# Linear attention, SoLU layer and top-2 experts on one core: expert slots split into 25 whole and six half ones

## The chip, the core and the metric

The kernel runs on one core of a Trainium2 chip. Its engines work side by side and wait for each other by semaphores: TensorE (PE, matrix products into the eight PSUM banks), VectorE (DVE), ScalarE (ACT), GpSimd (POOL, here mostly the issuer of indirect DMAs) and SyncE (SP, here the issuer of plain DMAs). The metric is the device time of one execution in microseconds (us), as the median of several runs.

## What is computed

Three stages, one after another, on 3072 tokens (4 batches of 768) with 384 features. This change touches the third only.

```python
attn_out = _attn_ref(q, k, v, a_re, a_im)          # decaying linear attention, 8 heads of 48
x = attn_out.transpose(0, 2, 1, 3).reshape(B * S, H * D)
x = _moe_ref(x, w_in, w_out, g_ln)                 # dense: 384 -> 1024, softmax gating, norm, -> 384
# _moe2_ref: E = 8 experts, each token goes to its two best
noisy_logits = x @ w_gate + np.log1p(np.exp(x @ w_noise)) * noise
top2, top2_w = two_largest(noisy_logits), softmax_of_the_two
for e in range(E):
    for k in range(2):
        mask = top2[:, k] == e
        h = np.maximum(x[mask] @ w1[e], 0.0)       # 384 -> 1024
        out[mask] += top2_w[mask, k, None] * (h @ w2[e])   # 1024 -> 384
```

## The kernel before

Up to about 600 us the first two stages run, tile by tile of 128 tokens, with the routing at their end. It writes the rows of x to `xs` in DRAM, and for each of the 6144 pairs (token, expert) a tag (row number, weight) to `tags`, sorted by expert: expert e has a region of its own.

The third stage works in **slots**. A slot is 256 rows of one expert (`CAP = 256`, two units of 128, `SUB = 2`). The number of slots is fixed when the program is built, `SLOTS = 31`, the most that eight experts can need. A small table, made on DVE in 14 chained steps while the last tags are written, says for each slot its expert and its first tag row (`slot_expert`, `slot_row`). A slot that gets no rows still does all its work on the engines, and its gathers and scatters move nothing.

Every product is made of three, from a high and a low part of both factors (`split_product`). So weights and tokens are first split: ACT casts the high part (`w1h`, `w2h`, `sxh`, `hh`), DVE subtracts it from the value for the low part (`w1l`, `w2l`, `sxl`, `hl`).

What a slot does, in the order that is written out for each engine, `s` being the slot:

- SP: `load_mine` (the tags of slot s + 3), then `load_w1` and `load_w2` (1.5 MB each, for slot s + 1) into the single buffers `raw1` and `raw2`. A load waits until DVE has made the low parts of the weights before it.
- POOL: `gather` (two indirect DMAs, the tokens of slot s + 2 into `xg`), `partial` (two more, the rows of `out` so far into `prev`), `give` (two more, the new rows into `out`). `partial` of a slot waits until the scatter of the slot before has landed.
- PE: eight blocks f. Each has `expert_hidden` of the next block (nine matmuls, w1 stationary, 256 tokens moving) and `expert_result` of this one (six matmuls, hidden rows stationary, 384 columns of w2 moving, accumulated over the eight blocks in the banks `Y_BANK`). In block 2 stand the six transposes of the next slot's tokens (`tokens`).
- ACT: the relu into `hh` of each block; in blocks 1 to 3 the casts of the next slot's w1 (`w1_piece`, three), in blocks 4 to 7 those of w2 (`w2_piece`, four), in block 4 the tokens.
- DVE: `hl` of each block and the low parts of the same pieces; in block 1 (`GIVE = 1`) the `give` of the slot before, `yo = bank * weight + prev`.

The order within an engine is the order of the program text; nothing reorders it. `apart` and `wait` are waits for semaphores.

Of the kernel before, what the change touches and what calls it, by code (L numbers as in the profile page):

```python
# [32 lines left out]
SLOTS = (2 * NTOK - (E - 1)) // CAP + E  # L33
# [11 lines left out]
LIVE = T - B  # L45
CHAIN = 3 * (LINE - 1)
# [4 lines left out]
LN_LIMIT = math.log(0.999)  # L51

# [35 lines left out]
def solu_moe_program(nc, q, k, v, a_re, a_im, w_in, w_out, g_ln, w_gate, w_noise, noise, w1, w2, out):  # L88
# [3 lines left out]
    with ExitStack() as ctx:  # L92
# [17 lines left out]
        tail_row = keep("tail_row", [1, E], I32)  # L110
        cnt = keep("cnt", [P, 4, E])
# [78 lines left out]
        thresh = m2("thresh", [P, E, MAXS])  # L190
        slot_no = m2("slot_no", [1, SLOTS, E])
        slot_cmp = m2("slot_cmp", [P, SLOTS, E])
        fills = m2("fills", [P, E, MAXS])
        assert m2.at <= early_end
        raw1 = m2("raw1", [P, KC, F])
        raw2 = m2("raw2", [P, FC, DM])
# [14 lines left out]
        prev = [m2(f"prev{i}", [P, SUB, DM]) for i in range(2)]  # L211
        bank = psum("bank", [P, 8, 512])
# [82 lines left out]
        raw1_loaded = sem("raw1_loaded")  # L295
        raw2_loaded = sem("raw2_loaded")
# [8 lines left out]
        h2_mm = sem("h2_mm")  # L305
        hh_done = sem("hh_done")
# [13 lines left out]
        turned = bank[:, 4:6, :].rearrange("p b x -> p (b x)")[:, 0:KC * CAP]  # L320

# [59 lines left out]

        def over_slots(eng, body):

            body(0, 0, True)
            body(1, 1, True)
            with eng.Fori(1, SLOTS // 2) as i:
                body(2 * i, 0, True)
                body(2 * i + 1, 1, True)
            for s in range(SLOTS // 2 * 2, SLOTS):
                body(s, s % 2, s < SLOTS - 1)  # L390
# [24 lines left out]
        def _(sp):  # L415
# [78 lines left out]
            def body(c, b, n):  # L494
# [6 lines left out]
                if n == T:  # L501
                    prepared(sp)
                    sp.dma_start(raw1[:], w1[0:1].rearrange("e (c p) f -> p (e c) f", p=P)).then_inc(raw1_loaded, 16)
                    sp.dma_start(raw2[:], w2[0:1].rearrange("e (c p) d -> p (e c) d", p=P)).then_inc(raw2_loaded, 16)
# [10 lines left out]
            def load_w1(s):  # L515
                e = sp.value_load(slot_expert[0:1, bass.ds(s, 1)], min_val=0, max_val=E - 1)
                apart(sp, (w1_lo, KC * s))
                sp.dma_start(raw1[:], w1[bass.ds(e, 1)].rearrange("e (c p) f -> p (e c) f", p=P)).then_inc(raw1_loaded, 16)

            def load_w2(s):  # L520
                e = sp.value_load(slot_expert[0:1, bass.ds(s, 1)], min_val=0, max_val=E - 1)
                apart(sp, (w2_lo, W2P * s))
                sp.dma_start(raw2[:], w2[bass.ds(e, 1)].rearrange("e (c p) d -> p (e c) d", p=P)).then_inc(raw2_loaded, 16)

            def load_mine(s, k):
                row = sp.value_load(slot_row[0:1, bass.ds(s, 1)], min_val=0, max_val=ROWS - CAP)
                apart(sp, (y_sent, 32 * (s - NM + 1)))
                sp.dma_start(mine[k][:].rearrange("p s i -> p (s i)"),
                             tags[bass.ds(row, CAP)].rearrange("(p s) i -> p (s i)", s=SUB)).then_inc(mine_loaded[k], 16)
# [5 lines left out]
            sp.wait_ge(slot_step, 14)  # L535
# [10 lines left out]
            sp.wait_ge(y_sent, 32 * SLOTS)  # L546
# [3 lines left out]
        def _(pool):  # L550
# [72 lines left out]
            def body(c, b, n):  # L623
# [16 lines left out]
                if n == T:  # L640
# [4 lines left out]
                    nc.gpsimd.iota(slot_no[:], [[1, SLOTS], [0, E]], base=0, channel_multiplier=0,  # L645
                                   allow_small_or_imprecise_dtypes=True).then_inc(tables_ready, 1)
                    nc.gpsimd.iota(thresh[:], [[0, E], [CAP, MAXS]], base=0, channel_multiplier=0,
# [67 lines left out]
        def _(act):  # L715
# [267 lines left out]
            for s_ in range(SLOTS):  # L983
                slot(s_, s_ % 2, s_ < SLOTS - 1)
# [692 lines left out]
```

## Time and profile before

| | us |
|---|---|
| median of 3 runs | 1179.63 (1179.08 to 1182.27) |
| the profiled execution | 1182.65, with a span of 1180.9 |
| mean granted TensorE clock over the span | 0.944 of full speed |

The profile comes from one execution. Its times are counted from the start of its span; the difference between the execution's time and its span lies outside of all engines' work. Start times and durations of single instructions overlap a little where an engine is pipelined: a matmul's duration is about 0.17 us longer than its distance to the next.

### The profile page before, as it was taken

What the parts mean: (1) busy time and instruction counts of PE and PEld (TensorE: products, weight loads), DVE (VectorE), ACT (ScalarE), POOL (GpSimd) and SP (SyncE); (2) the same over time, 40 slices, a digit from 0 to 9 for tenths busy, and PEclk for the clock granted to TensorE, in tenths of its full rate; (3) what the DMA queues carried; (4) which work ended last, traced back from release to release, by engine and by line L of the source; (5) the groups of instructions that cost most, each with busy time, mean ns of one, the idle gap of its engine ahead of it and who ended that gap; (6) DMA issues with size and microseconds to landing.
All of it is one profiled execution on the core that took longest, in us unless ns stands there. A gap on an engine that the chain in (4) does not pass through costs nothing.

```text
span 1180.9 us, 21982 instructions
## 1 busy us (share of the span) xinstructions
PE 1046.8 (89%) x7898; PEld 983.2 (83%) x7898; DVE 857.6 (73%) x1592; ACT 647.9 (55%) x1105; POOL 459.4 (39%) x413
## 2 busy tenths in 40 slices
PE   0467789989999999999939999999999999999996
PEld 0256678877887888888739999999999999999995
DVE  5799788988888899646445777676676676676672
ACT  6733856756756745645524555555555555555551
POOL 4011233344444443434531443453453453454342
PEclk9868888989999999999968999999999999999998
DMA  9430121231221211222216667676676676776740
GB/s 260 152 101 21 41 88 31 65 88 28 68 89 28 68 36 54 49 55 64 98 28 246 230 210 266 237 234 237 229 254 247 238 246 214 237 256 206 231 142 1
DMA packets 85980, 167.51 MB, mean 142 GB/s; under 512 B 18566, under 2 KB 57696, under 8 KB 85872
## 3 DMA queue, kind: packets, MB, share of 16 engines
q1 hardware_dynamic: 72336, 137.61, 36.3%
q0 software_dynamic: 13440, 28.40, 6.5%
q8 instruction: 63, 1.03, 0.4%
q14 instruction: 45, 0.37, 0.1%
q10 hardware_dynamic: 96, 0.10, 0.0%
HBM read 148.83 MB, written 21.92 MB: 145 GB/s over the span
## 4 chain that ended last, share of the span: by engine, by line
PE 59%; DVE 2%; ACT 1%; issue 1%; DMA 1%; POOL 0%; POOLq 0%; DVEq 0%; ACTq 0%; SPq 0%
PE bank L1412 23%; PE bank L1609 22%; PE bank L1473 4%; PE bank L1521 4%; PE bank L1403 3%; PE bank L1495 1%; PE bank L1533 1%; ACT z L943 1%; ACT x2t L938 0%; PE bank L1510 0%; DVE w1l L1145 0%; DMA xg<-xs,mine 0%; DMA tags<-tag,idx 0%; DVE zl L1247 0%; PE bank L1553 0%
## 5 line engine op out<-in xcount | busy, mean ns | idle before, releaser
L975 ACT ACTIVATE hh<-bank 128x256 fp32r<-128x256 f32 x248 | 95.4, 385 | 256.3 <-PE bank L1412 256.3
L1412 PE MATMUL bank<-sxh,w1h 128*128 128x256 f32 x744 | 212.0, 285 | 2.1 <-DVE sxl L1362 2.1
L1412 PE MATMUL bank<-sxh,w1l 128*128 128x256 f32 x744 | 210.3, 283 | 0.0
L1412 PE MATMUL bank<-sxl,w1h 128*128 128x256 f32 x744 | 210.0, 282 | 0.0
L1381 DVE SCALAR_TENSOR_TENSOR hl<-bank,hh 128x256 fp32r<-128x256 f32 x248 | 105.0, 423 | 120.5 <-ACT hh L975 120.5
L697 POOL DMA_INDIRECT out<-yo,mine x62 | 77.5, 1250 | 279.0 <-DVE yo L1374 261.1
L1609 PE MATMUL bank<-w2h,hh 128*128 128x384 f32 x496 | 167.4, 337 | 0.0
L1609 PE MATMUL bank<-w2l,hh 128*128 128x384 f32 x496 | 166.8, 336 | 0.0
L1609 PE MATMUL bank<-w2h,hl 128*128 128x384 f32 x496 | 166.6, 336 | 0.0
L1412 PEld LDWEIGHTS bank<-sxh,w1h 128*128 128x128 f32 x744 | 140.8, 189 | 2.5 <-DVE sxl L1362 2.5
L1412 PEld LDWEIGHTS bank<-sxh,w1l 128*128 128x128 f32 x744 | 141.5, 190 | 0.0
L1412 PEld LDWEIGHTS bank<-sxl,w1h 128*128 128x128 f32 x744 | 141.0, 190 | 0.0
L1151 DVE TENSOR_TENSOR w2l<-raw,w2h 128x768 fp32r<-128x768 f32 x124 | 118.6, 958 | 27.8 <-ACT w2h L785 27.8
L1145 DVE TENSOR_TENSOR w1l<-raw,w1h 128x1024 fp32r<-128x1024 f32 x93 | 113.5, 1222 | 20.0 <-ACT w1h L780 16.7
L785 ACT ACTIVATE w2h<-raw 128x768 fp32r<-128x768 f32 x124 | 103.5, 837 | 0.0
L780 ACT ACTIVATE w1h<-raw 128x1024 fp32r<-128x1024 f32 x93 | 97.6, 1051 | 0.0
L676 POOL DMA_INDIRECT xg<-xs,mine x62 | 86.2, 1391 | 24.5 <-issue 17.4
L1609 PEld LDWEIGHTS bank<-w2h,hh 128*128 128x128 f32 x496 | 94.4, 190 | 0.2 <-DVE hl L1381 0.2
L1609 PEld LDWEIGHTS bank<-w2l,hh 128*128 128x128 f32 x496 | 94.4, 190 | 0.0
L1609 PEld LDWEIGHTS bank<-w2h,hl 128*128 128x128 f32 x496 | 93.4, 188 | 0.0
L1473 PE MATMUL bank<-wi_hi,xh 112*128 112x512 f32 x192 | 83.8, 436 | 5.7 <-issue 5.7
L688 POOL DMA_INDIRECT prev<-out,mine x62 | 74.1, 1195 | 22.1 <-issue 18.3
(202 smaller groups left out, 2328.4 us busy)
## 6 DMA issues: line engine op xcount, KB each, us to landing
raw<-in_w SPq DMA_DIRECT2D x62, 1536.0 KB, 7.6
ar<-in_a_re SPq DMA_DIRECT2D x6, 768.0 KB, 4.7
turn<-in_a_im SPq DMA_DIRECT2D x6, 768.0 KB, 5.9
qk<-in_q SPq DMA_DIRECT2D x48, 96.0 KB, 2.4
qk<-in_k SPq DMA_DIRECT2D x48, 96.0 KB, 2.5
out<-wide SPq DMA_DIRECT2D x9, 512.0 KB, 11.5
vt<-in_v SPq DMA_DIRECT2D x24, 192.0 KB, 2.7
xs<-x SPq DMA_DIRECT2D x24, 192.0 KB, 2.8
```

Of the source, the lines that this page charges most:

```text
L676: nc.gpsimd.indirect_dma_start(xg[par][:, u, :], None, xs, bass.IndirectOffsetOnAxis(ap=mine[k][:, u, 0:1], axis=0), bounds_check=NTOK - 1 ...
L688: nc.gpsimd.indirect_dma_start(prev[par][:, u, :], None, out, bass.IndirectOffsetOnAxis(ap=mine[k][:, u, 0:1], axis=0), bounds_check=NTOK ...
L697: nc.gpsimd.indirect_dma_start(out, bass.IndirectOffsetOnAxis(ap=mine[k][:, u, 0:1], axis=0), yo[par][:, u, :], None, bounds_check=NTOK - ...
L780: nc.scalar.activation(w1h[par][:, cc, :], raw1[:, cc, :], ACT.Copy).then_inc(w1_hi, 1)
L785: nc.scalar.activation(w2h[par][:, W2C * j:W2C * (j + 1), :], raw2[:, W2C * j:W2C * (j + 1), :], ACT.Copy).then_inc(w2_hi, 1)
L975: nc.scalar.activation(hh[:, f % NH, :], bank[:, f % 2, 0:CAP], ACT.Relu).then_inc(hh_done, 1)
L1145: V.tensor_tensor(w1l[par][:, cc, :], raw1[:, cc, :], w1h[par][:, cc, :].bitcast(F32), ALU.subtract).then_inc(w1_lo, 1)
L1151: V.tensor_tensor(w2l[par][:, cut, :], raw2[:, cut, :], w2h[par][:, cut, :].bitcast(F32), ALU.subtract).then_inc(w2_lo, 1)
L1381: V.scalar_tensor_tensor(out=hl[:, f % NH, :], in0=bank[:, f % 2, 0:CAP], scalar=0.0, in1=hh[:, f % NH, :].bitcast(F32), op0=ALU.max, op1= ...
L1412: ins = MM(dst, stationary[a_](cc), moving[b_](cc), start=(n_ == 0), stop=(n_ == len(terms) - 1))
L1473: ins = MM(bank[:, 4 + half, :], (xh, xl)[a_][0:PR, cc, :], (wi_hi, wi_lo)[b_][0:PR, cc, 512 * half:512 * half + 512], start=(k_ % (3 * NP ...
L1609: ins = MM(bank[:, Y_BANK[par] + u, 0:DM], a_[:, f % NH, rows], b_[par][:, f, :], start=(f == 0 and k_ == 0), stop=(f == FC - 1 and k_ == 2))
```

## The change

The slots become 31 again, but of two sizes: 25 whole ones of 256 rows and six half ones of 128 rows, at places 3, 8, 13, 18, 23 and 28 of the list, so that two whole ones end it. An expert takes a whole slot for each 256 rows, another whole one for a rest over 128, and a half one for a rest of up to 128 rows; rests that find no half slot take whole ones from the end. The table gets longer for that, 24 chained steps on DVE and six more small tables (iota) on POOL.

A half slot has another form. Its tokens (128) are the stationary operand and w1 moves in two parts of 512 columns, so that the hidden rows come out one token to a partition; ACT's relu puts them into `row_h`, PE turns them in eight transposes into free banks, ACT and DVE make the high and low parts, and then the results follow, one unit instead of two.

The orders around it change: `raw1` and `raw2` get two buffers each and a load waits for the weights of two slots back; POOL reads `prev` first and then gathers for slot s + 3 instead of s + 2; the w1 pieces for the slot behind a half slot are made at the end of the slot before it; and the give stands in block 4 behind a half slot, then in blocks 3, 2 and 1.

```diff
-SLOTS = (2 * NTOK - (E - 1)) // CAP + E
+WHOLE, HALVES = 25, 6
+SLOTS = WHOLE + HALVES
+HALF_SLOTS = (3, 8, 13, 18, 23, 28)
...
+def give_block(s):
+
+    return max([GIVE] + [4 - (s - t) for t in HALF_SLOTS if t <= s])
...
 SP
             def load_w1(s):
-                apart(sp, (w1_lo, KC * s))
-                sp.dma_start(raw1[:], ...
+                apart(sp, (w1_lo, KC * (s - 1)))
+                sp.dma_start(raw1[s % 2][:], ...
...
 POOL
             for s in range(SLOTS):
-                if s + 2 < SLOTS:
-                    gather(s + 2, s % 2, (s + 2) % NM)
                 partial(s, s % 2, s % NM)
+                if s == 0:
+                    gather(2, 0, 2)
+                if s + 3 < SLOTS:
+                    gather(s + 3, (s + 3) % 2, (s + 3) % NM)
                 give(s, s % 2, s % NM)
...
 ACT, at the end of slot(s)
+                if is_half(s + 1) and s + 2 < SLOTS:
+                    for cc in range(KC):
+                        w1_piece(s + 2, par, cc)
...
+            def half_slot(s, par, more):
+                def row(part):
+                    act.wait_ge(h2_mm, s0 + part + 1)
+                    wait(act, row_turned, k - 1 + part)
+                    nc.scalar.activation(row_h[:, 512 * part:512 * (part + 1)], bank[:, part, :], ACT.Relu).then_inc(row_done, 1)
+                def high(part):
+                    act.wait_ge(row_turned, k + part + 1)
+                    act.wait_ge(y2_mm, s0 - 2 + 2 * part)
+                    nc.scalar.activation(hh_half[:, 4 * part:4 * (part + 1), :] ..., bank[:, turn_bank(par, part), :], ACT.Copy).then_inc(hh_done, 1)
+                row(0)
+                if more:
+                    tokens(s + 1, 1 - par)
+                row(1)
+                high(0)
+                high(1)
+                if more:
+                    for j_ in range(W2P):
+                        w2_piece(s + 1, 1 - par, j_)
...
 DVE
-                    if f == GIVE and s > 0:
+                    if s > 0 and f == give_block(s - 1):
                         give(s - 1, 1 - par, (s - 1) % NM)
...
 PE
+            def half_hidden(s, par, part):
+                if part == 0:
+                    pe.wait_ge(sx_lo, s + 1)
+                    pe.wait_ge(w1_lo, KC * (s + 1))
+                pe.wait_ge(hl_done, steps(s) - 1 + part)
+                cols = slice(512 * part, 512 * (part + 1))
+                split_product(bank[:, part, :],
+                              (lambda cc: sxh[par][:, cc, 0:P], lambda cc: sxl[par][:, cc, 0:P]),
+                              (lambda cc: w1h[par][:, cc, cols], lambda cc: w1l[par][:, cc, cols]), KC, h2_mm)
+            def half_turn(s, par, part):
+                pe.wait_ge(row_done, 2 * HALF_SLOTS.index(s) + part + 1)
+                for k_ in range(4):
+                    turn(bank[:, turn_bank(par, part), k_ * P:(k_ + 1) * P], row_h[:, ...], row_turned if k_ == 3 else None)
...
+            def half_slot(s, par, more):
+                if more:
+                    tokens(s + 1, 1 - par)
+                half_hidden(s, par, 1)
+                half_turn(s, par, 0)
+                half_turn(s, par, 1)
+                if more:
+                    first_hidden(s + 1, 1 - par)
+                half_result(s, par, 0)
+                half_result(s, par, 1)
```

How the instructions stand on DVE at the first half slot (slot 3), between the last block of slot 2 and the second block of slot 4; a name's last number tells buffers apart. Before, from the last two blocks of a slot on:

```order
L1151 TENSOR_TENSOR w2l_147<-raw_143,w2h_146 128x768
L1381 SCALAR_TENSOR_TENSOR hl<-bank,hh 128x256 x2
L1374 SCALAR_TENSOR_TENSOR yo_159<-bank,mine_65,prev_161 128x384 x2
L1145 TENSOR_TENSOR w1l_149<-raw_142,w1h_148 128x1024
L1381 SCALAR_TENSOR_TENSOR hl<-bank,hh 128x256
```

Of the change:

```order
L1236 TENSOR_TENSOR w2l_152<-raw_1_164,w2h_151 128x768
L1230 TENSOR_TENSOR w1l_146<-raw_0_143,w1h_145 128x1024 x3
L1471 TENSOR_TENSOR sxl_155<-bank,sxh_153 128x768
L1483 SCALAR_TENSOR_TENSOR yo_159<-bank,mine_61,prev_161 128x384 x2
L1509 TENSOR_TENSOR hl<-bank,hh 128x512 x2
L1236 TENSOR_TENSOR w2l_148<-raw_0_144,w2h_147 128x768 x4
L1490 SCALAR_TENSOR_TENSOR hl<-bank,hh 128x256 x2
```

Where one piece stood between two blocks, three w1 pieces, the tokens and the give of the slot before now stand in a row ahead of the half slot's two `hl`, and four w2 pieces behind them.

On ACT the same place reads, of the change:

```order
L832 ACTIVATE w2h_151<-raw_1_164 128x768
L827 ACTIVATE w1h_145<-raw_0_143 128x1024 x3
L1047 ACTIVATE row_h<-bank 128x512
L1016 ACTIVATE sxh_153<-bank 128x768
L1047 ACTIVATE row_h<-bank 128x512
L1052 ACTIVATE hh<-bank 128x512 x2
L832 ACTIVATE w2h_147<-raw_0_144 128x768 x4
L1029 ACTIVATE hh<-bank 128x256 x2
```

The three w1 casts stand ahead of the first relu of the half slot, where before one relu and one cast took turns.

On POOL, the last slots. Before:

```order
L676 DMA xg_66<-xs,mine_60 128x384 x2
L688 DMA prev_160<-out,mine_64 128x384 x2
L697 DMA out<-yo_158,mine_64 3072x384 x2
L688 DMA prev_161<-out,mine_65 128x384 x2
L697 DMA out<-yo_159,mine_65 3072x384 x2
L688 DMA prev_160<-out,mine_60 128x384 x2
L697 DMA out<-yo_158,mine_60 3072x384 x2
```

Of the change:

```order
L721 DMA xg_65<-xs,mine_59 128x384 x2
L742 DMA out<-yo_160,mine_62 3072x384 x2
L733 DMA prev_161<-out,mine_63 128x384
L742 DMA out<-yo_159,mine_63 3072x384
L733 DMA prev_162<-out,mine_64 128x384 x2
L742 DMA out<-yo_160,mine_64 3072x384 x2
L733 DMA prev_161<-out,mine_59 128x384 x2
L742 DMA out<-yo_159,mine_59 3072x384 x2
```

The last gather stands one slot earlier, and the third slot from the end moves one unit instead of two.

## Rows read from the trace of the kernel before

**Rows 1.** Busy time by stretches: start:end, length, then busy us (count) of each engine.

```profile
core 0: us, PE busy (x) PEld busy (x) DVE busy (x) ACT busy (x) POOL busy (x), PEclk, DMA share, GB/s
900.00:1000.00 100.00, 100.00 (x718) 99.83 (x718) 70.86 (x104) 54.19 (x92) 42.58 (x34) 1.00 0.71 246
```

**Rows 2.** Chain of waits, expert slots: start us, us, what.

```profile
739.12 1.07 PE bank L1412 x9
...
756.68 1.06 PE bank L1412 x9
...
1151.45 1.07 PE bank L1412 x9
1152.52 1.04 PE bank L1609 x6
1153.57 1.07 PE bank L1412 x9
```

**Rows 3.** Instructions in time, first phase: start, us, engine, line, [idle before, releaser].

```profile
521.75 0.40 PE L1473 MATMUL bank<-wi_lo,xh 112*128 112x512 f32 x1
...
526.74 0.39 PE L1473 MATMUL bank<-wi_hi,xl 112*128 112x512 f32 x1
...
527.17 1.23 DVE L1275 TENSOR_REDUCE nmax<-bank 128x1 f32<-128x1024 f32 x1 [3.26 <-PE bank L1473]
```

**Rows 4.** Groups by shape, 840 to 1120 and (last two) 300 to 560 us.

```profile
L1151 DVE TENSOR_TENSOR w2l<-raw,w2h 128x768 fp32r<-128x768 f32 x64 | 61.3, 958 | 14.8 <-ACT w2h L785 14.8
L1145 DVE TENSOR_TENSOR w1l<-raw,w1h 128x1024 fp32r<-128x1024 f32 x48 | 58.7, 1222 | 10.3 <-ACT w1h L780 8.3
L785 ACT ACTIVATE w2h<-raw 128x768 fp32r<-128x768 f32 x64 | 53.6, 837 | 0.0
L780 ACT ACTIVATE w1h<-raw 128x1024 fp32r<-128x1024 f32 x48 | 50.5, 1052 | 0.0
L1362 DVE TENSOR_TENSOR sxl<-bank,sxh 128x768 fp32r<-128x768 f32 x16 | 15.2, 951 | 0.0
...
L1312 DVE TENSOR_TENSOR xl<-bank,xh 112x512 fp32r<-112x512 f32 x13 | 8.9, 687 | 8.1 <-ACT xh L949 8.1
L949 ACT ACTIVATE xh<-bank 112x512 fp32r<-112x512 f32 x13 | 7.5, 577 | 0.0
```

**Rows 5.** A load of w1, its first cast, and the landing of all w1 loads.

```profile
898.32 0.38 SPq L518 DMA_DIRECT2D raw<-in_w  x1
...
909.11 1.05 ACT L780 ACTIVATE w1h<-raw 128x1024 fp32r<-128x1024 f32 x1
...
DMA to landing us min/median/max: 6.3/7.6/8.5
```

**Rows 6.** From give to give: DVE, POOL, and the landing of the reads of prev.

```profile
892.03 1.13 DVE L1374 SCALAR_TENSOR_TENSOR yo<-bank,mine,prev 128x384 f32<-128x384 f32 x2
...
895.50 1.35 POOL L697 DMA_INDIRECT out<-yo,mine  x1 [0.30 <-issue]
...
1144.61 1.05 POOL L688 DMA_INDIRECT prev<-out,mine  x1 [1.91 <-DMA out<-yo,mine]
...
DMA to landing us min/median/max: 3.9/5.0/5.7
```

**Rows 7.** The last two gives on DVE, of slots 29 and 30.

```profile
1155.43 1.13 DVE L1374 SCALAR_TENSOR_TENSOR yo<-bank,mine,prev 128x384 f32<-128x384 f32 x2
...
1169.60 1.14 DVE L1374 SCALAR_TENSOR_TENSOR yo<-bank,mine,prev 128x384 f32<-128x384 f32 x2 [1.41 <-PE bank L1609]
```

**Rows 8.** Between the phases: the first row lists loaded by table, DVE's first token part.

```profile
613.56 2.92 SPq L528 DMA_DIRECT2D mine<-tags  x3
...
621.77 0.96 DVE L1362 TENSOR_TENSOR sxl<-bank,sxh 128x768 fp32r<-128x768 f32 x1 [10.53 <-ACT sxh L966]
```

**Rows 9.** A pause of PE in the first phase, and the stretch behind it.

```profile
502.56 0.77 PE L1473 MATMUL bank<-wi_hi,xh 112*128 112x512 f32 x1 [1.35 <-issue]
...
502.00:505.70 3.70, 3.13 (x8) 2.52 (x9) 2.80 (x4) 1.51 (x3) 2.21 (x3) 0.55 0.39 24
```

More of the change, by code:

```diff
@@ L45 @@
 LIVE = T - B
+SLOT_STEPS = 24
 CHAIN = 3 * (LINE - 1)
@@ L51, with is_half, table_row, units @@
 LN_LIMIT = math.log(0.999)
+def is_half(s):
+    return s in HALF_SLOTS
+def table_row(s):
+    return WHOLE + HALF_SLOTS.index(s) if is_half(s) else s - sum(t < s for t in HALF_SLOTS)
+def units(s):
+    return 1 if is_half(s) else SUB
+def units_upto(s, step=1):
+    return sum(units(t) for t in range(s, -1, -step))
+def give_block(s):
+    return max([GIVE] + [4 - (s - t) for t in HALF_SLOTS if t <= s])
+def steps(s):
+    return sum(2 if is_half(t) else FC for t in range(s))
 def wait(eng, sem, value):
@@ L211, in solu_moe_program @@
         prev = [m2(f"prev{i}", [P, SUB, DM]) for i in range(2)]
+        raw1.append(m2("raw1_1", [P, KC, F]))
+        raw2.append(m2("raw2_1", [P, FC, DM]))
+        row_h = m2("row_h", [P, F])
         bank = psum("bank", [P, 8, 512])
@@ L674, in gather @@
                 wait(pool, sxt_mm, s - 1)
-                for u in range(SUB):
+                for u in range(units(s)):
                     nc.gpsimd.indirect_dma_start(xg[par][:, u, :], None, xs,
@@ L1337, in _, with over @@
             one = slice(0, 1)
-            count, slots, upto = cnt[:, 0, :], cnt[:, 1, :], cnt[:, 2, :]
+            count, whole, any_, odd, pairs_upto, odd_upto, odd_ahead = (cnt[:, i_, :] for i_ in range(7))
             by_slot = [1, SLOTS, E]
+            def over(x):
+                return x[one].unsqueeze(1).to_broadcast(by_slot)
             then(V.scalar_tensor_tensor(out=count, in0=expert_no[:], scalar=-float(REGION), in1=rank_base[:],
                                         op0=ALU.mult, op1=ALU.add))
-            then(V.tensor_tensor(fills[:], count.unsqueeze(2).to_broadcast([P, E, MAXS]), thresh[:], ALU.is_gt))
@@ L1357, in _ @@
-            then(V.tensor_copy(tail_row[:], rank_base[one]))
+            for i_ in range(2):
+                then(V.tensor_tensor(fills[:, i_], count.unsqueeze(2).to_broadcast([P, E, MAXS]), thresh[:, i_], ALU.is_gt))
+            then(V.tensor_reduce(cnt[:, 1:3, :], fills[:], AX.X, ALU.add))
+            then(V.tensor_tensor(odd, any_, whole, ALU.subtract))
+            then(V.tensor_tensor_scan(pairs_upto, ones[:, 0:E], whole, 0.0, ALU.mult, ALU.add))
+            then(V.tensor_tensor_scan(odd_upto, ones[:, 0:E], odd, 0.0, ALU.mult, ALU.add))
@@ new lines, in _ @@
+            then(V.tensor_tensor(odd_ahead, odd_upto, odd, ALU.subtract))
+            in_pairs, in_odd = (slot_cmp[:, i_] for i_ in range(2))
+            own = in_pairs
+            at_pair, at_odd = (x[:].unsqueeze(2).to_broadcast(by_slot) for x in (pair_no, odd_no))
+            then(V.tensor_tensor(in_pairs, over(pairs_upto), at_pair, ALU.is_le))
+            then(V.tensor_reduce(slot_f[:, 0, :], in_pairs, AX.X, ALU.add))
+            then(V.tensor_tensor(in_pairs, in_pairs, over(whole), ALU.mult))
```

250 lines of the change are left out of this document (163 added, 87 removed).

## The prediction, made before the changed kernel was timed

> **What bounds the kernel now.** I read in this order. First, the busy time by stretches: in 900 to 1000 us TensorE (PE) is busy for all 100 us at the full granted clock, while VectorE (DVE) has 71 us of work, ScalarE (ACT) 54 us and the DMA engines a share of 0.71 [rows 1]. So in the expert phase, about 622 to 1170 us, PE alone sets the pace and a matmul less is time less. Second, the chain of waits. The same block of nine matmuls stands at 739.12 and at 756.68, one slot later: a slot of 256 rows costs **17.56 us**. A hidden block starts at 1151.45 and its result block at 1152.52, the next hidden block at 1153.57: nine matmuls of 256 columns are 1.07 us (0.118 each), six of 384 columns 1.05 us (0.175 each) [rows 2]. Eight such pairs are 16.9 us; the remaining 0.66 us are the six transposes of the next slot's tokens, 0.11 us each. There are 31 such slots, 544 us.
>
> **What a half slot costs PE.** 31 slots stay 31, but six of them hold 128 rows. In a half slot the tokens are the stationary operand and w1 moves 512 columns at a time: 2 parts of 9 matmuls. The only rows of that width are those of the first phase, 22 steps from 521.75 to 526.74, 0.227 us each, with 112 partitions instead of 128 [rows 3]; I take that value, since the columns, not the partitions, should count. 18 x 0.227 = 4.09. The hidden rows must then be turned: 8 transposes x 0.11 = 0.88. The result is 8 blocks of 3 matmuls of 384 columns: 24 x 0.175 = 4.20. Its own tokens: 3 x 0.11 = 0.33. Sum **9.50 us** of PE work, 8.06 less than a whole slot.
>
> **What PE waits for in a half slot.** Take 0 at the start of the first hidden part; this walk uses PE's order of the change. Part 0 ends at 2.04, the last result block of the slot before at 3.09, the next slot's six transposes at 3.75, part 1 at 5.79. Turn 0 needs row_h part 0. ACT does three w1 casts before it (3 x 1.05, and rows overlap by about 0.1) and the copy of 512 columns (0.58) [rows 4]: done near 3.6, 2.2 us before it is wanted. Turn 0 runs 5.79 to 6.23. Turn 1 needs row_h part 1: a reader of a bank starts 0.2 us after PE's last matmul has made way (DVE at 527.17, against 526.74 + 0.23) [rows 3], so ACT runs 5.99 to 6.57, and PE starts at about 6.60: **0.37 us idle**. Turn 1 ends at 7.04, and PE covers with the next slot's first hidden block until 8.10. Meanwhile ACT copies turned part 0 (behind the row, to 7.1) and DVE subtracts it, 0.69 [rows 4], to 7.8; the result needs it at 8.10. Part 1 follows at 7.8 on ACT and 8.5 on DVE; wanted at 10.2. DVE ahead of that has three w1 pieces (1.22 each), the tokens (0.95) and two gives (1.13 together) [rows 4, 6], from about 1.2: free at about 6.9, 0.3 before it is needed. So in total 9.50 + 0.37 = 9.87, and six half slots save 6 x (17.56 - 9.87) = **46.1 us**. The wait is bounded by 0 and by the chain with nothing beside it (0.2 + 0.58 + 0.44 + 0.2 + 0.58 + 0.69 = 2.7, and 0.44 for the other turn: 3.1 us). I take 0.37, the walk, because ACT and DVE are free in it; the bounds are +2.2 and -17 us on the saving.
>
> One rule prices the matmuls otherwise. The Trainium skill ("TensorE: Matmul & The Clock Gate", section Back-to-back issue gap) gives columns divided by 2.4 GHz plus 2.5 ns. By that 512 columns would take 0.216 us, 384 0.163, 256 0.109 and 128 0.056, and the same sum would save about 43 us instead of 46; the rows disagree with it by 5 to 8% (0.227, 0.175, 0.118), and I use the rows.
>
> **The whole slots around.** In the slot before a half one ACT and DVE get three w1 pieces more, at its end, and in the half slot four w2 pieces. Their sum over five slots is unchanged except for turns, and both have slack in a stretch (29 and 46 us in 100) [rows 1]. After the half slot ACT has the four w2 casts (4 x 0.84) behind it before the next relu, and DVE 4 x 0.96 [rows 4]: DVE is through at 12.4, then the first hl block until 12.7; PE wants it at 13.4 (end of the results 12.3, then a hidden block). No price; without this 0.7 us, PE waits for the difference.
>
> **Weights and tokens.** raw1 and raw2 are doubled, so a load waits for the weights two slots back instead of one. Before, w1 is issued at 898.32 and its first cast starts at 909.11, 10.8 us later, and landing takes 6.3 to 8.5 us [rows 5]. Now a pair is asked for a slot earlier, so a half slot's short time is covered. The bytes of weights stay as they are, 31 pairs, in 46 us less: DMA share from 0.71 to about 0.77. Cost nothing; if it did, a cast would be late. Gathers go a slot earlier too and stand behind the read of prev on POOL: no path.
>
> **The chain from one give to the next.** give on DVE, scatter, its landing, read of prev, landing, next give. From the give at 892.03 to the end of the second scatter issue, 895.50 + 1.35, are 4.8 us; the read of prev can start 1.9 us after that (at 1144.61 it waited 1.91 for the scatter), its second issue 1.3 later, and that lands after 5.0 (3.9 to 5.7) [rows 6]: 13.0 us. In the middle gives are 15.4 us apart (17.56 less a block of 2.11): nothing. At the **end** it shows. Two whole slots end the list, and the give of slot 29 moves from block 1 of slot 30 to block 3: 4.2 us later. Today it starts at 1155.43 and the last give at 1169.60, when PE is done [rows 7], 14.2 us later. Now that gap is 14.2 - 4.2 = 10.0 us, and the chain asks for 13.0 (11.9 with the shortest landing): PE is done and the last give waits **2 to 3 us**. I take 2.8.
>
> **Between the phases.** DVE's table is 24 chained steps instead of 14. Before, they end at 611.24, since DVE idles 10.53 us before 621.77 [rows 8]; even with 0.5 us for each of the ten more they end by 616.3: covered. I reckon with 4 us, 615.2. SP waits for the table with the load of the row lists: first such load at 613.56 [rows 8], now about 615.4, and everything behind it on SP (the weights of slot 1) 1.8 us later; slot 1's weights are wanted only behind the first hidden blocks of slot 0. POOL builds six small tables more. All told 0 to 1 us, taken as 0.5.
>
> **Sum.** The profiled execution took 1182.65 us (span 1180.9), the median of the runs is 1179.63, 3.0 lower. 1182.65 - 46.1 + 2.8 + 0.5 = 1139.9; on the scale of the median **1136.8, rounded 1137**, 3.6% faster.
>
> **Rivals.**
> A. The narrow chain stands open: bank reads, turns and DVE in series, 3.1 us in each half slot instead of 0.37. 6 x 2.7 = 16: 1153. For it: DVE is free only 0.3 us before it is needed. Against: each link is short and PE has a block to put between. With half of it, 1145. Chance 0.11.
> B. The clock falls in half slots. In the first phase PE idles 1.35 us before 502.56, and in the 3.7 us around and behind it the mean granted clock is 0.55, close to the 1.2 GHz level, 1.7 us lost [rows 9]. Six times 1.7 is 10: 1147. Against: the idle time here is 0.37, a quarter of that. Chance 0.08. This is also where the Trainium skill speaks against the change: the same page, section Part 4: PE-mode transpose, says that transposes do not count as activity for the full clock as matmuls do, and the half slot adds eight of them to the pause; by that rule B is the outcome. The six token transposes of today's slots cost no clock in 100 us [rows 1], but they stand in no pause.
> C. Slower. The chain of gives becomes the pace. It decides from where 13.0 us turns into more than 17.56, for instance if scatters and reads land 2.5 us later each under the extra weight traffic (18.1): then 31 x 18.1 = 561 us against 544 now, **1197**. Against: measured landings spread by 1.8 us only, and the traffic rises by a tenth. Chance 0.03.
> D. The change does not pay what it says: the half slots take a whole slot's time because a load is late (8 us in each): 1180 to 1183. Against: the loads start a slot earlier. Chance 0.02.
>
> **Numbers.** Forecast 0.73 (1131 to 1143); A 0.11, B 0.08, C 0.03, D 0.02; better than 1131, with no wait at all and cheaper turns, 0.03. The range 1131 to 1148 holds the forecast, B and the smaller half of A. About 0.3%, 3.5 us, is what a measurement can tell here from no change; faster than that 0.95, same 0.02, slower 0.03.
>
> **What would show it.** The slot's period in the chain of waits stays 17.56 us for whole slots; half slots add 9.9 us. PE idles once in each, before the second turn, for row_h, 0.3 to 0.5 us; a longer idle behind DVE hl is A. The granted clock stays 1.00 through the phase, else B. The last yo waits for prev by DMA, 2 to 3 us. Weight casts never wait for raw. The forecast fails if matmuls of 512 columns with tokens stationary take more than 0.24 us, or if any wait in a half slot passes 1.5 us.

## The result, and the profile of the changed kernel

| | us | ratio to before |
|---|---|---|
| before, median of 4 runs | 1179.78 (1179.08 to 1182.27) | |
| changed, median of 4 runs | 1151.34 (1145.31 to 1153.23) | 0.974 (0.971 to 0.976) |
| forecast | 1137 (1131 to 1148) | |

Faster by 2.6%, where 3.6% was forecast: the direction is right, the time is 14 us too long and above the range. The profiled execution took 1149.61 us, with a span of 1147.9 and a mean granted clock of 0.939.

Busy time of the changed kernel by stretches (start:end, length, busy us and count of PE, PEld, DVE, ACT, POOL, granted clock, DMA share, GB/s). It answers to [rows 1]:

```profile
700.00:800.00 100.00, 98.05 (x685) 96.42 (x684) 71.66 (x102) 56.02 (x93) 41.00 (x34) 1.00 0.72 252
...
900.00:1000.00 100.00, 98.61 (x687) 96.80 (x686) 71.80 (x103) 55.80 (x92) 38.99 (x34) 1.00 0.71 249
1000.00:1100.00 100.00, 93.70 (x631) 90.93 (x631) 69.27 (x96) 55.30 (x90) 36.55 (x31) 0.98 0.69 242
```

PE was busy for 100 of 100 us before. Now it has holes, small ones up to 1000 us and 6.3 us of them in the last stretch, where the clock falls once as well. What it waits for is in the table of waits, 620 to 1140 us (engine, line, releaser: us in total, times, longest):

```profile
POOL prev L733 <- DMA out<-yo,mine: 85.0, 29, 6.2
...
DVE yo L1483 <- DMA prev<-out,mine: 16.4, 9, 5.3
...
PE bank L1745 <- DVE hl L1490: 8.6, 7, 4.7
...
PEld bank L1745 <- DVE hl L1490: 2.4, 4, 1.3
```

Read from the bottom: PE waits for `hl`. DVE is late with `hl` since it stood in a give, waiting for the read of `prev`. And that read can't leave before the scatter in front of it has landed, for which POOL waits 29 times. Before, over 700 to 1170 us, a read waited for a scatter twice, 3.8 us in all, DVE never for `prev` and PE's matmuls never for `hl`. The number of POOL's waits is mostly its new order: before, two gathers filled that time, and the read left 3.8 us behind the end of the scatter's issue (900.63 against 895.50 + 1.35), where it now leaves after 2.5. What has grown is the landing, below. This is the chain of gives, the path on which the prediction put "nothing".

The chain of waits of the changed kernel runs through it (start us, us, what):

```profile
713.96 1.14 DVE yo L1483 x2
...
717.43 3.16 DMA out<-yo,mine
...
723.54 7.34 DMA prev<-out,mine
...
731.01 1.15 DVE yo L1483 x2
...
739.45 7.94 DMA prev<-out,mine
...
747.52 1.15 DVE yo L1483 x2
```

From give to give are 17.05 and 16.51 us. The first of them: give to second scatter issue 3.5, its landing and the restart of POOL 4.0 (717.43 to the read at 721.42), from the first read's issue to the second's 2.1, and the landing 7.3 (7.9 in the next). PE's pace wants 15.4 here. PE feels it two DVE instructions later, and most at 1080 us (instructions in time; in brackets the idle time before and its releaser):

```profile
750.28 0.41 PE L1745 MATMUL bank<-w2h,hh 128*128 128x384 f32 x1 [1.53 <-DVE hl L1490]
...
1080.02 0.66 PE L1745 MATMUL bank<-w2h,hh 128*128 128x384 f32 x1 [4.73 <-DVE hl L1490]
```

Which transfer stands beside it shows on SP and POOL together. SP, then POOL, of the changed kernel, 720 to 726 us:

```profile
720.81 0.35 SPq L564 DMA_DIRECT2D mine<-tags  x1
721.98 0.38 SPq L554 DMA_DIRECT2D raw<-in_w  x1
724.66 0.38 SPq L559 DMA_DIRECT2D raw<-in_w  x1
```

```profile
721.42 1.82 POOL L733 DMA_INDIRECT prev<-out,mine  x1 [2.45 <-DMA out<-yo,mine]
723.54 1.77 POOL L733 DMA_INDIRECT prev<-out,mine  x1 [0.30 <-issue]
```

The first SP line is `load_mine`, the other two are the loads of w1 and w2. `load_mine` waits for the scatter whose row list it overwrites. w1's doubled buffer is free by then, and w1 leaves 1.2 us behind it. w2's is let go by the last `w2l` on DVE, which here ends at 724.43:

```profile
723.47 0.96 DVE L1236 TENSOR_TENSOR w2l<-raw,w2h 128x768 fp32r<-128x768 f32 x1 [0.31 <-ACT w2h L832]
```

So w1 and w2, 1.5 MB each, leave in the 4 us behind the scatter's landing, together with the read of `prev`. Before, w1 left at 898.32, ahead of the read (900.63, 901.94), and w2 at 906.95, after it had landed, 8.6 us apart instead of 2.7: the single buffers had paced them (SP waited for `w1l` 26 times and for `w2l` 27 times over 640 to 1100 us, and never for a scatter; now it waits for the scatter 25 times). In most slots of the changed kernel w2 leaves between 1.2 and 6.5 us behind w1. Landings of the reads over 640 to 1100 us, to be held against [rows 6] (3.9/5.1/5.8 in this stretch before):

```profile
DMA to landing us min/median/max: 4.4/6.8/8.2
```

In the last two of SP's 30 rounds there is no `load_mine` left, and its wait is gone with it. In the first of them w1 leaves in front of the scatter's landing. SP, then POOL:

```profile
1061.54 0.38 SPq L554 DMA_DIRECT2D raw<-in_w  x1
```

```profile
1059.55 1.20 POOL L742 DMA_INDIRECT out<-yo,mine  x1 [7.28 <-DVE yo L1483]
1061.05 1.14 POOL L742 DMA_INDIRECT out<-yo,mine  x1 [0.31 <-issue]
1068.34 1.57 POOL L733 DMA_INDIRECT prev<-out,mine  x1 [6.15 <-DMA out<-yo,mine]
```

The wait for the scatter is 6.15 us instead of 2.44: the give that follows, at 1077.27, is 19.7 us behind the one before it, and PE pays the 4.73 us above.

The half slot itself does what the walk said. Chain of waits, slot 3 of the changed kernel:

```profile
677.85 2.08 PE bank L1544 x9
679.94 1.06 PE bank L1745 x6
681.00 0.66 PE bank L1535 x6
681.65 2.09 PE bank L1544 x9
...
683.76 0.61 ACT row_h L1047
...
684.42 0.66 PE bank L1535 x4
685.07 1.07 PE bank L1544 x9
686.15 4.17 PE bank L1773 x24
690.31 1.07 PE bank L1544 x9
```

The walk put 12.30 us from the first hidden part to the second hidden block of the next slot (690.31 here); it took 12.46.

### The profile page after: what moved, and what is told of

Its sections match the earlier page's. It is cut to its first block, busy times and chain, and to the rows that moved or that the text cites. A ratio compares the mean times of both kernels' runs of the same rounds, so it can differ in the third digit from the quotient of the medians.

```text
span 1147.9 us, 20986 instructions
## 1 busy us (share of the span) xinstructions
PE 1005.0 (88%) x7460; PEld 932.9 (81%) x7460; DVE 846.1 (74%) x1560; ACT 640.4 (56%) x1081; POOL 423.1 (37%) x401
## 4 chain that ended last, share of the span: by engine, by line
PE 40%; DMA 10%; issue 5%; DVE 4%; ACT 2%; POOL 1%; POOLq 0%; DVEq 0%; ACTq 0%; SPq 0%
PE bank L1544 13%; PE bank L1745 11%; DMA prev<-out,mine 7%; PE bank L1605 4%; PE bank L1653 4%; DMA out<-yo,mine 3%; PE bank L1535 3%; PE bank L1773 2%; DVE yo L1483 1%; PE bank L1627 1%; PE bank L1665 1%; DVE w1l L1230 1%; ACT z L990 1%; POOL out L742 0%; POOL prev L733 0%
## 5 line engine op out<-in xcount | busy, mean ns | idle before, releaser
L1544 PE MATMUL bank<-sxh,w1h 128*128 128x256 f32 x600 | 171.9, 287 | 2.1 <-DVE sxl L1471 2.1
L1544 PE MATMUL bank<-sxh,w1l 128*128 128x256 f32 x600 | 169.8, 283 | 0.0
L1544 PE MATMUL bank<-sxl,w1h 128*128 128x256 f32 x600 | 169.6, 283 | 0.0
L1745 PE MATMUL bank<-w2h,hh 128*128 128x384 f32 x400 | 136.1, 340 | 8.8 <-DVE hl L1490 8.6
L1745 PE MATMUL bank<-w2l,hh 128*128 128x384 f32 x400 | 134.8, 337 | 0.0
L1745 PE MATMUL bank<-w2h,hl 128*128 128x384 f32 x400 | 134.7, 337 | 0.0
L1544 PEld LDWEIGHTS bank<-sxh,w1h 128*128 128x128 f32 x600 | 113.7, 190 | 2.5 <-DVE sxl L1471 2.5
L1544 PEld LDWEIGHTS bank<-sxh,w1l 128*128 128x128 f32 x600 | 114.4, 191 | 0.0
L1605 PE MATMUL bank<-wi_lo,xh 112*128 112x512 f32 x192 | 81.0, 422 | 0.0
L1605 PE MATMUL bank<-wi_hi,xl 112*128 112x512 f32 x192 | 80.0, 417 | 0.0
```

The lines of the kernel that those rows point to most:

```text
L1544: ins = MM(dst, stationary[a_](cc), moving[b_](cc), start=(n_ == 0), stop=(n_ == len(terms) - 1))
L1605: ins = MM(bank[:, 4 + half, :], (xh, xl)[a_][0:PR, cc, :], (wi_hi, wi_lo)[b_][0:PR, cc, 512 * half:512 * half + 512], start=(k_ % (3 * NP ...
L1745: ins = MM(bank[:, Y_BANK[par] + u, 0:DM], a_[:, f % NH, rows], b_[par][:, f, :], start=(f == 0 and k_ == 0), stop=(f == FC - 1 and k_ == 2))
```

## The experiments

Each ratio below is to the kernel before, run on the same chip, with its 95% interval.

The theory after the comparison: the chain from give to give has grown from 13 us to 16 or 17, since its read of `prev` lands beside the weight loads, and over the cycle of a half slot and four whole ones (9.87 + 4 x 17.56 = 80.1 us for five gives) only 16.0 us each are there. The rivals: the half slots are dearer than reckoned (and the chain only a symptom); POOL's new order is the cause; the longer table; the doubled buffers alone.

### The chain out of the way

Changed kernel, and the kernel before with the same edit:

```diff
-                wait(pool, y_sent, 16 * units_upto(s - 1))
                 wait(pool, y2_evac, units_upto(s - 2))
...
-  nc.gpsimd.indirect_dma_start(prev[par][:, u, :], None, out, ...
+  nc.gpsimd.indirect_dma_start(prev[par][:, u, :], None, xs, ...
...
+                wait(pool, y_sent, 16 * units_upto(s - 1))
                 pool.wait_ge(y2_evac, units_upto(s))
```

> The changed kernel, but prev is read from xs instead of out and that read waits for no scatter (the scatters wait for each other instead); the outputs lack the sums over an expert's partners. Same traffic, same work on every engine, only the chain give, scatter, read, give is open. If that chain is what ate the gain (7 waits of PE for hl behind a late yo, 8.6 us, and one clock fall behind them): 1137 to 1141 us, no PE wait for hl longer than 0.2 us. If the half slots themselves cost more than reckoned, or the weights' traffic does: it stays at 1148 to 1152.

> The kernel before with the same edit (prev from xs, no wait for the scatter; sums left out in the same way). Its slots are 17.56 us apart and the chain is shorter, so nothing waits for it: 1179 to 1181, as before. The difference to the changed kernel with the same edit is then the bare price of six half slots against whole ones: 46 us by my sum less about 1 to 2 us at the start of the phase, so 43 to 46.

Measured: the changed kernel 1136.52 us (1134.08 to 1142.02), ratio 0.961 (0.956 to 0.966); the one before 1181.28, ratio 1.000 (0.998 to 1.003), against 1181.35 for before on this chip. Without the chain the six half slots are worth 1181.28 - 1136.52 = 44.8 us, against 46.1 in the sum. So the half slots are not dear, and the chain, which cost nothing before, now holds about 15 us (1151.34 - 1136.52 = 14.8, on two chips). Busy time of the changed kernel with this edit:

```profile
900.00:1000.00 100.00, 99.75 (x699) 98.49 (x698) 73.18 (x104) 57.24 (x96) 42.69 (x35) 1.00 0.75 257
1000.00:1100.00 100.00, 99.50 (x682) 97.13 (x681) 75.28 (x103) 60.27 (x96) 37.38 (x30) 1.00 0.67 235
```

PE is whole again but for 0.25 us in a half slot, no clock falls, and nothing waits for `hl` longer than 0.2 us. Both loads still run, at a DMA share of 0.75: the traffic alone, without the chain, costs nothing.

### What makes the chain longer

First POOL's order, the one of before put back:

```diff
+                if s + 2 < SLOTS:
+                    gather(s + 2, s % 2, (s + 2) % NM)
                 partial(s, s % 2, s % NM)
-                if s == 0:
-                    gather(2, 0, 2)
-                if s + 3 < SLOTS:
-                    gather(s + 3, (s + 3) % 2, (s + 3) % NM)
                 give(s, s % 2, s % NM)
```

> The changed kernel with POOL's order of before: gather for slot s + 2, then the read of prev. Theory one (weights in front of the read): the read is issued some 2.6 us later and behind two gathers, but the scatter's landing is hidden by them; net chain about 0.5 us longer, 1150 to 1156. Theory two (gathers behind the read slow it): the landing falls to 5 us and the time to 1144 or less.

Measured: 1150.99 us, 0.972 (0.968 to 0.976), no different from the change. The gathers now fill POOL's wait (POOL waited for the scatter 13.9 us in all instead of 85.0), but the read still lands after 6.6 us, and DVE waits 19.2 us for it. The order on POOL is not the cause.

Then the same loads at other times. The weights asked for ahead of the row list's wait:

```diff
+                load_w1(s + 1)
+                load_w2(s + 1)
                 if s + 3 < SLOTS:
                     load_mine(s + 3, (s + 3) % NM)
-                load_w1(s + 1)
-                load_w2(s + 1)
```

> The changed kernel, SP asks for the weights of slot s + 1 ahead of the row list of slot s + 3, so that the two loads no longer leave together right when a scatter has landed, which is also when prev is read. Theory one, the read of prev lands late (6.7 us median against 5.0) because 3 MB of weights are in front of it: landing back at about 5, 1139 to 1144. Theory two, it lands late because the order on POOL changed (gathers behind it): no change, 1148 to 1152.

Measured: 1179.2 us, 0.998 (0.996 to 1.000): all of the gain gone, where a better time was expected. Its waits, 620 to 1140 us:

```profile
POOL prev L733 <- DMA out<-yo,mine: 120.4, 27, 6.6
...
DVE yo L1483 <- DMA prev<-out,mine: 41.7, 11, 5.3
PE bank L1745 <- DVE hl L1490: 30.8, 11, 4.7
```

The read did get quicker, 5.8 us in the middle, but w1 now leaves at 714.24, between the two scatters (713.70 and 715.22), and the scatter pays:

```profile
722.92 1.04 POOL L733 DMA_INDIRECT prev<-out,mine  x1 [6.17 <-DMA out<-yo,mine]
```

And w2 held back until the read of two slots before has landed:

```diff
                 load_w1(s + 1)
+                if s >= 2:
+                    sp.wait_ge(prev_loaded[(s - 2) % 2], 16 * units_upto(s - 2, 2))
                 load_w2(s + 1)
```

> The changed kernel, but SP asks for w2 of slot s + 1 only when the read of prev of slot s - 2 has landed; w1 stays where it is. The run with the weights ahead of the row list showed that the scatter (6.2 us at its worst) suffers just as the read does when a load stands in front of it. If any transfer of the chain is late by what is loaded beside it, then one load beside the read is what the kernel before had: read landing back to about 5.0 to 5.5 us, scatter at 2.5, 1138 to 1144. If it's not the loads, the read stays at 6.7 and the time at 1148 to 1152; if w2 now falls on the scatter instead, 1150 or more.

Measured: 1173.64 us, 0.991 (0.989 to 0.993); a miss of the same kind. Behind the read's landing comes the give, so w2 (707.08) now leaves just ahead of the next scatter (707.87), which waits 6.07 us. POOL's waits for the scatter rise to 133.5 us, PE's for `hl` to 23.1. With the give put ahead of the tokens in the half slot on top of it:

```diff
+                give(s - 1, 1 - par, (s - 1) % NM)
                 if more:
                     tokens(s + 1, 1 - par)
-                give(s - 1, 1 - par, (s - 1) % NM)
                 low(0)
```

> As the run with w2 after the read, and in a half slot DVE gives the slot before ahead of splitting the tokens, so that the give of that slot starts 1.1 us sooner and the chain of five slots has 81.2 instead of 80.1 us. If the chain still binds in some slots: 0.5 to 1.5 us less than that run; if it is free there: the same.

Measured: 1172.38 us, 0.990 (0.988 to 0.993). The intervals of the two overlap: a microsecond on DVE gains nothing that is measured. In the kernel without it two gives of most cycles are 17.3 to 17.7 us apart, where the same two are 15.5 us apart with the chain out of the way.

So a load of 1.5 MB lengthens whatever small indirect transfer it is asked for just before or beside: the scatter by about 3.7 us (6.1 against 2.4), the read by 2 to 3 in the middle. If it is the bytes that do it, loading only an eighth of them from slot 2 on, with every wait and issue in its place, must heal all:

```diff
-  sp.dma_start(raw1[s % 2][:], w1[...])
+  sp.dma_start(raw1[s % 2][:, :, 0:128 if s > 1 else F], w1[...][:, :, 0:128 if s > 1 else F])
...
-  sp.dma_start(raw2[s % 2][:], w2[...])
+  sp.dma_start(raw2[s % 2][:, 0:1 if s > 1 else FC, :], w2[...][:, 0:1 if s > 1 else FC, :])
```

> The changed kernel with an eighth of the weights loaded from slot 2 on (the rest of the buffers keeps the weights of slots 0 and 1, so the outputs are those of wrong weights; all work on the engines and the whole chain of gives stay). If the loads beside them are what makes scatter and read late: the read lands after 3.5 to 4 us, the scatter is waited for 2 us, no wait of yo for prev but the last, 1135 to 1139. If the chain is late by itself (issues on POOL, rows of DRAM, gathers behind it): the read stays above 6 us and the time at 1147 to 1152.

Measured: 1137.73 us, 0.962 (0.959 to 0.965), as without the chain, and 12.4 us less than the changed kernel on the same chip (1150.13, below). Waits of this kernel, 620 to 1140 us:

```profile
POOL prev L733 <- DMA out<-yo,mine: 71.1, 29, 3.4
...
DVE yo L1483 <- DMA prev<-out,mine: 1.8, 1, 1.8
```

Two gives of it stand at 710.59 and 726.05, 15.46 us apart, PE's own pace, where the changed kernel takes 16.5 to 17.1 with the same waits. The scatter that w1 runs beside in the last rounds is waited for 3.4 us, not 6.15. Its trace has no landings of the reads, so the 3.5 to 4 us that were expected stay unread; that DVE waits for `prev` only once stands in their place. The weight bytes beside the chain are the cause, shown: the bytes without the chain cost nothing, nor does the chain without the bytes.

Not all of the chain's growth is theirs. POOL of this kernel, the same place:

```profile
718.05 1.82 POOL L733 DMA_INDIRECT prev<-out,mine  x1 [2.45 <-DMA out<-yo,mine]
720.18 1.78 POOL L733 DMA_INDIRECT prev<-out,mine  x1 [0.30 <-issue]
```

The 2.45 us behind the scatter and the 2.1 us from the first read's issue to the second's stand here too, with small loads; they belong to the chain itself, at this place. What the bytes add is the landing of the read and, now and then, that of the scatter (its waits are 85.0 us in 29 against 71.1 in 29).

### The doubled buffers, and the table, alone

The kernel before with two `raw1` and `raw2` and its loads a slot earlier:

```diff
-                apart(sp, (w1_lo, KC * s))
-                sp.dma_start(raw1[:], ...
+                apart(sp, (w1_lo, KC * (s - 1)))
+                sp.dma_start(raw1[s % 2][:], ...
```

> The kernel before with the doubled raw1 and raw2 and the loads two slots back, nothing else. Theory: its loads now leave together when a scatter has landed, so the read of prev lands at 6.5 to 7 us instead of 5.0; but its gives are 17.56 us apart and the time stays at 1180 to 1183. If the landing stays at 5.0, POOL's new order or the half slots made it late, not the loads.

Measured: 1183.81 us, 1.001 (0.999 to 1.003) against 1183.01. The time doesn't move; there the chain has 17.56 us. On the landing it settles nothing, since the landings of the reads are missing in its trace. But it shows what bunches the loads: here w1 leaves at 703.93 and w2 only at 710.87. SP and DVE:

```profile
710.87 0.38 SPq L525 DMA_DIRECT2D raw<-in_w  x1
```

```profile
709.67 0.96 DVE L1153 TENSOR_TENSOR w2l<-raw,w2h 128x768 fp32r<-128x768 f32 x1 [0.31 <-ACT w2h L787]
```

w1 follows the scatter's landing as in the changed kernel, and w2 follows the last `w2l` as there; but the give stands in block 1, so the scatter lands about 8 us before that `w2l` ends. With the give in a later block, as in the changed kernel, the two releases fall together. So the doubled buffers alone don't bunch the loads; the later give is needed as well. (The later give with single buffers was not run.)

The kernel before with six more small tables and ten more chained steps:

```diff
+                    for i_ in range(3):
+                        for a_, b_ in ((0, 25), (25, 31)):
+                            nc.gpsimd.iota(slot_f[:, 5 + i_, a_:b_], ...
...
+            for _ in range(6):
+                then(V.tensor_tensor(cmp1, slot_no[:], slot_no[:], ALU.mult))
+            for _ in range(4):
+                then(V.tensor_scalar(slot_f[:, 5, :], slot_f[:, 6, :], 1.0, None, ALU.mult))
```

> The kernel before with six more small iotas on POOL and ten more chained steps in the table on DVE (idle work, thrown away). The changed kernel's first tokens were turned at 620.54 us instead of 619.20. If the tables make that, this runs 1.3 us longer than before (1182 to 1183); if it is a difference between executions of the first phase, 0 to 0.5.

Measured: 1185.69 us, 1.002 (1.000 to 1.003): at most 0.3%, and the interval just includes no change. Its profile shows the table done at 619.2 and the first tokens turned at 624.66, 5.5 us later than before; but the table's first step was 4.8 us late already (612.01 against 607.24), so at most 0.7 us are left for the table in this trace.

### A better version, and the change once more

What the last two rounds cost can be had back by one wait: the row list's wait, kept where no row list is left to load.

```diff
                 if s + 3 < SLOTS:
                     load_mine(s + 3, (s + 3) % NM)
+                else:
+                    sp.wait_ge(y_sent, 16 * units_upto(s - 3))
                 load_w1(s + 1)
```

> The changed kernel; in the last three rounds of SP's list, where no row list is left to load, the wait that stood in front of it (scatter of slot s - 3 landed) is kept, so that no weights start beside that scatter. In the changed kernel a w1 load issued at 1061.54 stood in front of the scatter of 1059.55 to 1062.2, which was then waited for 6.15 us instead of 2.44, PE lost 4.73 us to it and the clock fell once after (1.7 us). Theory: those 5 to 6.5 us come back, 1142 to 1147 where the changed kernel again has 1149 to 1152. If that one event was chance, no difference.

The same with the give ahead of the tokens in half slots (the edit shown above):

> As the run before, and in a half slot DVE gives ahead of splitting the next tokens, 1.1 us sooner. The chain of five gives has then 81.2 us instead of 80.1 for five links of 16 to 16.5: the waits of 0.3 to 1.5 us in front of the half slots shrink. 1 to 3 us less than that run, 1139 to 1145; if the later tokens hold up PE's first block of the next slot instead, the same or slower.

The changed kernel unaltered, on the same chip:

> The changed kernel as it is, beside the others on the same chip: 1147 to 1153. It shows how far its waits move between executions; the end's 6 us wait for a scatter should be there again.

Measured: 1145.02 (1142.63 to 1146.5), 0.967 (0.964 to 0.970); 1145.55, 0.968 (0.965 to 0.971); and 1150.13 (1149.47 to 1153.57), 0.971 (0.969 to 0.974). The wait of the last two rounds (two, not the three of the expectation) is worth 5 us. POOL of the gated kernel, then of the changed one again:

```profile
1062.28 1.14 POOL L744 DMA_INDIRECT out<-yo,mine  x1 [0.31 <-issue]
1065.86 1.08 POOL L735 DMA_INDIRECT prev<-out,mine  x1 [2.44 <-DMA out<-yo,mine]
```

```profile
1063.85 1.14 POOL L742 DMA_INDIRECT out<-yo,mine  x1 [0.31 <-issue]
1071.30 1.40 POOL L733 DMA_INDIRECT prev<-out,mine  x1 [6.32 <-DMA out<-yo,mine]
```

So the 6 us wait is no accident of one execution. The gated kernel is the fastest here that does all the work, together with the one that gives earlier, which can't be told from it; its PE still waits 6.4 us for `hl` in six places of up to 2.4 us. The earlier give takes that to 4.4 us and gains nothing that is measured, where 1 to 3 us were expected.

## Why the prediction was right, and where it failed

**What a half slot costs: right.** Six half slots against whole ones were put at 46.1 us; with the chain out of the way the difference of two kernels is 44.8. Nine matmuls of 512 columns take 2.08 and 2.09 us (forecast 2.04), the 24 of the result 4.17 (4.20), and the walk of 12.30 us came out 12.46, so the true term was about 45. One row of matmuls with 112 partitions [rows 3] was a fair price for 128. The Trainium skill ("TensorE: Matmul & The Clock Gate", section Back-to-back issue gap) has columns divided by 2.4 GHz plus 2.5 ns; an estimate by it is 1.94 us for such nine, 7% short of the trace, as with the rows of before.

**PE idles once in a half slot, before the second turn: right.** PE, first half slot; the same 0.25 us stands in all six:

```profile
684.42 0.66 PE L1535 MATMUL bank<-ident,row_h 128*128 128x128 f32 x4 [0.25 <-ACT row_h L1047]
```

With the part of a matmul that the trace still shows as busy, about 0.4 us of the chain, 0.37 forecast. On DVE, the low parts were in time although three pieces, the tokens and the gives stand ahead of them, and no result block of a half slot waited. Rival A was not seen. Nor did the whole slots around cost anything: with the chain out of the way nothing waited for `hl` longer than 0.2 us.

**No clock falls in half slots: right.** It stayed at 1.00 through the stretches above up to 1000 us. The one fall stands behind the 4.7 us wait (start:end, then as above):

```profile
1076.00:1080.00 4.00, 0.00 (x0) 0.01 (x1) 2.73 (x5) 0.66 (x1) 0.76 (x1) 0.94 0.32 117
1080.00:1083.40 3.40, 3.38 (x14) 3.30 (x15) 2.47 (x3) 0.00 (x0) 1.57 (x2) 0.57 0.31 116
1083.40:1090.00 6.60, 6.60 (x50) 6.60 (x49) 4.22 (x7) 3.74 (x7) 4.45 (x4) 1.00 0.83 298
```

Nothing for 4 us, then 3.4 us at 0.57, close to the 1.2 GHz level, 1.5 us lost, then full speed. It is a consequence of the chain, not of the half slots. What the Trainium skill says of transposes (same page, section Part 4: PE-mode transpose), that they don't count as busy in the same way, didn't decide here: eight of them around a pause of 0.25 us, six times, cost no clock.

**"In the middle gives are 15.4 us apart: nothing": this step failed.** The chain was summed to 13.0 us from a kernel in which nothing pressed it. Its terms in the changed kernel: the start of the read behind the scatter 2.45 us instead of 1.9, the second issue up to 2.1 instead of 1.3, and the landing 6.8 in the middle and up to 8.2 instead of 5.0. That is 16 to 17 us (measured 16.51 and 17.05), over the 15.4 between two gives and even over the mean of 16.0. The first two terms, 1.4 us, were mis-sized: the 1.9 was read at 1144.61, where the kernel ends, and with small loads both stay as they are in the changed kernel. The third, 2 to 3 us, is what the weight loads do. With the first two alone the chain is 14.4 us, under 15.4, and costs nothing, as the run with small loads shows; the third takes it over. The bound that was given, 5.7, was the largest landing of before, that is of a kernel whose single buffers kept w2 off the read.

**"Weights and tokens ... Cost nothing": the step behind it.** It asked only whether a load comes in time for its casts, and there it held: casts waited for `raw` 0.3 us in all. It didn't ask beside what the load now runs. The DMA share that was named, 0.77, wasn't even reached (0.71 to 0.72): the mean traffic hardly rose, its place moved. The loads' own landings stretched as well, over 640 to 1100 us from 7.6 in the middle and 8.2 at most to 8.4 and 13.1, without harm.

**Rival C, with a chance of 0.03, had the mechanism and the wrong threshold.** It was to decide "from where 13.0 us turns into more than 17.56"; but a give moved by a block per slot has 15.4 us, and a cycle with a half slot in it 80.1 / 5 = 16.0. Its price went with that: not 31 times the excess, but about a microsecond in some of the slots, and 5 us in one at the end.

**The end: mis-sized.** 2.8 us were taken; the last give came 10.6 us behind the one before it, against 10.0 without any wait. DVE and POOL:

```profile
1127.54 1.13 DVE L1483 SCALAR_TENSOR_TENSOR yo<-bank,mine,prev 128x384 f32<-128x384 f32 x2
...
1138.12 1.14 DVE L1483 SCALAR_TENSOR_TENSOR yo<-bank,mine,prev 128x384 f32<-128x384 f32 x2 [2.04 <-DMA prev<-out,mine]
```

```profile
1135.89 1.01 POOL L733 DMA_INDIRECT prev<-out,mine  x1 [0.31 <-issue]
```

The read issued at 1135.89 landed 2.1 us later, not 5.0. No weights are loaded any more at the end, and this read moved nothing (0 GB/s over 1135 to 1140 us); which of the two makes it short isn't told apart. PE's last matmul ended at 1137.46, and before, the last give began 0.04 us behind PE; here 0.66, so the wait is worth 0.6 us.

**Between the phases: about right.** The table's steps run from 608.48 to 616.07, 7.6 us, and the row lists leave at 617.13 instead of 613.56 [rows 8]. The first tokens are turned 1.3 us later than before, 0.5 forecast. But the table's first step stood at 607.24 before, so 1.2 us of the 1.3 lie ahead of the table; and in the other kernels of this study that moment lay anywhere between 616.29 and 628.47. So it is mostly a difference between executions of the first phase; 0.1 us is what the table can have cost.

**The account.** Expert phase, from the first hidden block to the end of PE: 513.3 us (624.13 to 1137.46) against 546.8, 33.5 saved where 46.1 were forecast. Of the 12.6 missing, 8.6 are PE's waits for `hl`, 1.5 the clock, 1.0 the half slots (six times 0.16), and 1.5 are not told apart (weight loads of PE also waited for `hl`, 2.4 us in all, partly in the same places). The start adds 0.8, the last give takes off 2.2, and 1.5 more go behind it: from the end of the last scatter's issue to the end of the span are 5.5 us instead of 7.0, for no reason that the trace shows. That makes 9.7 us, and the profiled execution is 9.8 behind the sum, 1149.61 against 1139.85. The other 4.7 us of the 14.5 are scale: the sum was taken 3.0 us down because before's profiled execution lay above its median, and that of the changed kernel lies 1.7 below its own.

**What stays open.** That the weight bytes do it is shown, in what way isn't: no run tells whether the indirect transfer stands behind the load in a queue, or shares bandwidth with it. Neither of the two other orders of SP keeps the loads apart from both the scatter and the read, as the single buffers of before did; 7 to 9 us are left between the gated kernel (1145.0) and the two without the conflict (1136.5 and 1137.7).

## What to carry to other kernels

Before slots are shortened, take the chain that runs through memory from one to the next (scatter, landing, read, landing) and hold it against the shortest distance that it will have, not against the old period; its landings are those of the old neighbourhood of transfers. A deeper buffer doesn't only let a load come earlier, it lets go of what timed it: look which wait the load then follows, and which small transfer leaves in the same microseconds. Here that wait was for a scatter, and the scatter moved when the give was put into a later block; the doubled buffers alone, in the kernel before, cost nothing. And where a loop's last rounds skip an instruction, they skip its wait too.

## What the runs showed of the hardware

- An indirect scatter of 128 rows lets its waiter go 2.44 us after the end of its issue, time and again, with large and with small loads around. With a plain load of 1.5 MB asked for within 1 us of the issue it takes 5.9 to 6.6 us (changed kernel, in both of its traces, and the two other orders of SP). Asked for 2 to 4 us ahead of the issue, the load makes it 3.5 to 6.4 us (the two other orders), and 6 to 9 us ahead 2.4 to 4.3 us (changed kernel). With an eighth of the bytes, 0.7 us behind the issue, it takes 3.4 us.
- An indirect read of 128 rows of 1.5 KB landed after 5.0 us in the middle beside the tail of one load (before), after 6.8 (up to 8.2) with w1 asked for 0.6 us behind the first read's issue and w2 within 1 to 6 us of it, after 3.7 when it left ahead of both (of `xs`, with the chain out of the way), and after 2.1 when it moved nothing and no load ran.
- Over 640 to 1100 us two loads of 1.5 MB that left 8.6 us apart landed after 7.6 us in the middle and 8.2 at most; mostly leaving 1.2 to 6.5 us apart, after 8.4 and 13.1, at the same mean share of the DMA engines (0.71).
